# Moving the gate's work within the instruction order of ScalarE and VectorE in an attention, mixture-of-experts and dense kernel

## The reference

```
scores = x @ state.T / 8 ; xread = softmax(scores) @ state      # attention, both ways
sread  = softmax(state @ x.T / 8) @ x
x = rows of concat(xread, sread)                                # 8 * (512 + 32) = 4352 rows of 512
xn = x / (norm(x) + 1e-6) ; en = emb / (norm(emb) + 1e-6)
logits = xn @ en.T / tau ; e = argmax(logits)                   # one expert for each row
gate = softmax(logits)[e]
x = gate * (relu(x @ w1[e]) @ w2[e])
h = relu(x @ w_in) ; out = (s * h * h + b) @ w_out              # dense stage
```

## Time and profile before

| | |
|---|---|
| median of three runs | 1475.15 us |
| the profiled execution's own time | 1475.15 us |
| its span, first to last instruction | 1473.5 us |
| mean granted TensorE clock | 0.966 of full speed |
| TensorE busy | 1366.4 us, 93% |
| VectorE busy | 661.5 us, 45% |
| ScalarE busy | 511.6 us, 35% |
| GpSimd busy | 157.4 us, 11% |

### The profile page before, as it was taken

One profiled execution on the slowest core, in us unless ns is written; L12 is line 12 of the kernel. 1 busy time (PEld: TensorE's weight loads), 2 busy tenths in 40 slices (PEclk: granted clock), 3 DMA queues, 4 the chain that ended last, 5 costly groups with the idle time before them and its releaser, 6 DMA issues.

```text
span 1473.5 us, 22797 instructions
## 1 busy us (share of the span) xinstructions
PE 1366.4 (93%) x6879; PEld 1124.7 (76%) x6880; DVE 661.5 (45%) x1680; ACT 511.6 (35%) x977; POOL 157.4 (11%) x200
## 2 busy tenths in 40 slices
PE   3788668999999999998999999999999999999995
PEld 2555556888888887886888888888888888888884
DVE  2777653466765477466532322323233232422422
ACT  2555322455554355353422222222222222222221
POOL 1122220011110011015000100101001010100101
PEclk8888798999999999998999999999999999999998
DMA  8354325144423144123110000101001010010000
GB/s 218 90 123 94 73 47 187 47 172 172 172 101 115 44 171 156 61 69 125 37 43 1 29 29 0 57 0 57 0 0 57 0 57 0 23 34 0 29 0 29
DMA packets 75490, 100.21 MB, mean 68 GB/s; under 512 B 44312, under 2 KB 44856, under 8 KB 74432
## 3 DMA queue, kind: packets, MB, share of 16 engines
q1 hardware_dynamic: 62784, 69.72, 15.7%
q0 software_dynamic: 7200, 20.08, 4.1%
q10 hardware_dynamic: 5472, 9.96, 1.8%
HBM read 71.24 MB, written 28.66 MB: 68 GB/s over the span
## 4 chain that ended last, share of the span: by engine, by line
PE 80%; DVE 7%; DMA 3%; issue 3%; ACT 3%; SPq 2%; DVEq 1%; ACTq 0%; another core or an unknown queue 0%; POOL 0%; POOLq 0%
PE bank_a L1450 25%; PE bank_n L1469 13%; PE bank_t L1469 12%; PE bank_n L1403 11%; PE bank_a L1372 9%; DMA xg<-x_tok,g_idx 3%; PE bank_t L1383 2%; DVE w_lo L963 1%; PE bank_t L1190 1%; PE bank_n L1354 1%; PE bank_a L1261 1%; PE bank_n L1261 1%; PE bank_a L1173 1%; ACT x_rows L595 1%; PE bank_n L1231 1%
## 5 line engine op out<-in xcount | busy, mean ns | idle before, releaser
L1125 DVE TENSOR_TENSOR sq<-rel 128x512 f32<-128x512 f32 (+1 forms) x144 | 95.5, 663 | 487.1 <-ACT rel L764 487.1
L764 ACT ACTIVATE rel<-bank_a 128x512 f32<-128x512 f32 (+1 forms) x144 | 82.8, 575 | 541.6 <-PE bank_a L1450 541.6
L1450 PE MATMUL bank_a<-y_hi,w_in_hi 128*128 128x512 f32 (+1 forms) x576 | 217.7, 378 | 0.1
L1450 PE MATMUL bank_a<-y_hi,w_in_lo 128*128 128x512 f32 (+1 forms) x576 | 217.3, 377 | 0.0
L1450 PE MATMUL bank_a<-y_lo,w_in_hi 128*128 128x512 f32 (+1 forms) x576 | 217.3, 377 | 0.0
L1403 PE MATMUL bank_n<-w_hi,hid_hi 128*128 128x512 f32 x296 | 118.9, 402 | 16.0 <-DVE hid_lo L979 15.6
L1450 PEld LDWEIGHTS bank_a<-y_hi,w_in_hi 128*128 128x128 f32 x576 | 108.3, 188 | 21.4 <-issue 0.8
L1450 PEld LDWEIGHTS bank_a<-y_lo,w_in_hi 128*128 128x128 f32 x576 | 108.3, 188 | 20.7 <-issue 0.2
L1450 PEld LDWEIGHTS bank_a<-y_hi,w_in_lo 128*128 128x128 f32 x576 | 108.3, 188 | 19.9
L1403 PE MATMUL bank_n<-w_hi,hid_lo 128*128 128x512 f32 x296 | 117.7, 398 | 0.0
L1469 PE MATMUL bank_n<-wo_hi,g_hi 128*128 128x512 f32 x288 | 112.5, 391 | 0.7 <-DVE g_lo L1128 0.7
(11 more groups left out here) (231 smaller groups left out, 2121.2 us busy)
## 6 DMA issues: line engine op xcount, KB each, us to landing
w_raw<-in_moe_w SPq DMA_DIRECT2D x16, 2048.0 KB, 9.4
moe_tok<-yg ACTq DMA_DIRECT2D x38, 256.0 KB, 2.0
x_tok<-x_rows SPq DMA_DIRECT2D x8, 1088.0 KB
x_m<-in_x SPq DMA_DIRECT2D x8, 1024.0 KB
y_rows<-moe_tok SPq DMA_DIRECT2D x8, 1024.0 KB, 5.1
win_raw<-in_moe_w_in SPq DMA_DIRECT2D x8, 512.0 KB
w_raw<-in_moe_w_out SPq DMA_DIRECT2D x1, 4096.0 KB
slot_tab<-ids,pos POOLq DMA_INDIRECT x40
```

Source lines behind the costliest of these rows:

```text
L764: nc.scalar.activation(rel[:, k, 0:cols], ps_g[k][:, 0:cols], ACT.Relu).then_inc(rel_ready, 1)
L1125: nc.vector.tensor_tensor(sq[:, 0:cols], rel[:, k, 0:cols], rel[:, k, 0:cols], ALU.mult).then_inc(sq_ready, 1)
L1450: last = nc.tensor.matmul(ps_g[n % 2][:, 0:cols], w[:, wc], a[:, c, 0:cols], start=(c == 0 and w is w_in_hi and a is y_hi), stop=(c == DC ...
```

## The change

Only the order of calls changes. On ScalarE `gate_square(1)` is called before `hidden(0)`, `gate_soft(0)` after `next_w1(1)`, `gate_square(3)` before `hidden(2)`, `gate_square(4)` before `win_hi(0)`; in the loop `next_w1` comes before `gate_square`. On VectorE the gate of tiles 0 and 1 comes after `hidden_lo(1)`; in the loop `gate_scale` comes before `next_w1`, and `gate_logits` moves from before `next_w1` to behind `hidden_lo`.

```diff
 (scalar)
             x_hi(0)
             gate_square(0)
+            gate_square(1)
             hidden(0)
             x_hi(1)
             hidden_hi(0)
-            gate_square(1)
             hidden(1)
-            gate_soft(0)
             hidden_hi(1)
+            act.wait_ge(st_stored, 16 * B)
             act.wait_ge(tab_ready, 1)
             next_w1(1)
-            act.wait_ge(st_stored, 16 * B)
+            gate_soft(0)
             result(0)
...
             gate_soft(2)
+            gate_square(3)
             hidden(2)
             x_hi(3)
-            gate_square(3)
             next_w1(2)
             hidden_hi(2)
+            gate_square(4)
             win_hi(0)
             next_w2(1)
-            gate_square(4)
             gate_soft(3)
...
                 x_hi(g + 2)
+                next_w1(g + 1)
                 gate_square(g + 3)
-                next_w1(g + 1)
                 result(g)
 (vector)
-            gate_scale(0)
             dve.wait_ge(slot_tr, 1)
             nc.vector.tensor_copy(idx_all[:], bank_r[:, E:E + 3 * TQ]).then_inc(idx_ready, 1)
-            gate_final(0)
-            gate_scale(1)
             hidden_lo(1)
             dve.wait_ge(tab_ready, 1)
             next_w1(1)
+            gate_scale(0)
+            gate_final(0)
             x_lo(2)
             gate_logits(2)
+            gate_scale(1)
             gate_final(1)
             gate_scale(2)
+            gate_logits(3)
             gate_final(2)
             x_lo(3)
-            gate_logits(3)
+            gate_scale(3)
             next_w1(2)
             hidden_lo(2)
+            gate_logits(4)
             win_lo(0)
             next_w2(1)
-            gate_logits(4)
-            gate_scale(3)
             gate_final(3)
...
                 x_lo(g + 2)
+                gate_scale(g + 2)
+                next_w1(g + 1)
+                hidden_lo(g + 1)
                 gate_logits(g + 3)
-                next_w1(g + 1)
-                gate_scale(g + 2)
-                hidden_lo(g + 1)
                 next_w2(g)
                 gate_final(g + 2)
```

## The result

The changed kernel takes 1490.75 us (median of 4 runs, 1487.78 to 1493.85), the kernel before 1474.63 on the same chip: a ratio of 1.0108, with a 95% interval of 1.0084 to 1.0132. It is slower by 16.1 us. The forecast was 1494.

A forecast was written before the change was run, and what follows sets the result against it. TensorE, busy 93% of the span, bounds the kernel. The loop loses 17.1 us (24.3 after, 7.2 before), the start 1.0 and the last gathers 0.4: +18.5 on 1475.15, called 1494, range 1477 to 1508.

The forecast's parts named there:

- likeliest case: Whole kernel: TensorE stalls 2.0 us on the gather at six changes of expert, 1.0 more follows each; 1494 us, chance 0.50.
- VectorE's sum at a change: Loop, change of expert: gate_scale ahead of w1_lo, which ends at T + 11.9; TensorE loses about 0.9 us instead of 0.44.
- T: The end of up(g + 1) on TensorE, from which the forecast counts times in the loop.
- signs of being wrong: Profile after: no gather wait at L1354 in the loop, a w1_lo wait at L1372, or plain tiles longer than 12.25 us.
- The gather's lateness: Loop, change of expert: the gather waits for logits behind hidden_lo and is issued at T + 14.4.
- The load in its way: Loop, six changes: the gather, 2.4 us behind the w1 load, takes 7.0 us; TensorE stalls 2.0 us.
- the cover: Loop: the gather's margin before TensorE needs it, 0.45 us at worst in a plain tile, gone at a change.
- What is late next: After each of six stalls: x_lo about 0.6 us late, hidden_lo some 0.5; 1.0 us taken, bounds 0 and 1.7.
- The other bound, the clock: Behind each stall: TensorE's granted clock falls, worth 1.7 us each; as a rival 1502 us in all, chance 0.15.
- The gather under `w_out`: Last gathers, under the 4 MB load of w_out: 0.4 us lost, bounds 0 and 1.
- The start: Ahead of the loop: ScalarE waits for gather 1, up(1) comes about 2.4 us later; +1.0 us, bounds -1 and +2.
- The end of the loop: Loop's end: the gate's chain and hidden_lo keep their sum, so it costs nothing.

The follow-up runs named there:

- Experiment 6: Kernel before with only VectorE's gate_scale moved ahead of next_w1 in the loop: 1476.31 us against 1475.72, ratio 1.0016.
- experiment 4: Changed kernel with the loop's w1 loads fetching only half the rows, output wrong: 1466.78 us against 1466.59 for the kernel before, ratio 1.0001.
- experiment 1: Changed kernel with gate_logits moved back right behind x_lo in VectorE's loop: 1468.64 us against 1466.59 for the kernel before, ratio 1.0002.
- experiment 2: Kernel before with only gate_logits moved behind hidden_lo in VectorE's loop: 1482.60 us against 1466.59, ratio 1.0110.
- experiment 3: Kernel before with only the changed order of calls ahead of the loops, on both engines: 1465.76 us against 1466.59, ratio 0.9991.
- experiment 7: Kernel before with ScalarE's next_w1 ahead of gate_square and GpSimd's bias sum moved behind the last gate: 1471.98 us against 1475.72, ratio 0.9979.

## Why the prediction was right

The prediction's likeliest case came true, in its direction, its place and nearly its size.

- *VectorE's sum at a change.* Forecast: `w1_lo` ends and the w1 load goes at T + 11.95. It goes at T + 11.96. The loss of 0.9 us for it shows by itself at the seventh change: 0.96. Experiment 6 shows it is real and small. One of the signs of being wrong did come: seven waits at `up` for the last quarter of `w1_lo`, which I had ready just in time. They are 0.2 us each and lie inside the 0.96.
- *The gather's lateness.* Forecast: issue at T + 14.4 at a change. It is T + 14.16, and GpSimd's wait is put down to the logits 36 times.
- *The load in its way.* Shown: the gather takes 6.28 us, with half the load it takes no longer than with none, and the loss is gone (experiment 4); issued well ahead of the load it does no harm (experiment 1). I took 7.0 us; the six measured 6.13 to 6.30. The gather lands with the end of the load; in my sum both stood at T + 21.4, though I had the 7.0 from other rows. The 9.4 us that I took for the load is the median of a group that has the w2 loads in it as well; the w1 loads behind which the six gathers come take 8.3 to 8.7. The gather's time was 0.7 us too large and its issue 0.2 too late, so TensorE's idle time is 0.76 to 0.98 us and not 2.0.
- *What I read wrongly in the trace before.* I had today's gather out of the load's way because it is issued ahead of it. At 296.79 it is only 0.6 us ahead (the load goes at 297.40), and it is held up already. GpSimd's timeline in the trace before:

```profile
305.33 0.18 POOL L512 COPY g_idx<-idx_all 128x1 int32 x1 [7.11 <-DMA xg<-x_tok,g_idx]
```

  Its landing is seen 7.11 us after the issuing instruction's end, instead of some 3.2. It costs nothing there, since TensorE wants it only near 308 us. So the change did not bring the gather and the load together at this change of expert; it moved both later, and that used up the cover.
- *A cost that I left out.* Behind that idle time, the transposes and the start of `up` are some 0.6 to 0.8 us slower than in a row: `up` starts 0.99 us behind `turn_x` (306.53 to 307.52), 0.36 in other tiles, a third of a microsecond of it as "issue". TensorE's own register loads for the expert's number stand there, and with a full queue they would be covered; that reading of it was only argued. Idle time and this together give 1.7 us (2.67, the mean cost in the spacing over a change, less 0.96), where the forecast had 2.0. That the two come near each other is luck: the wait was taken twice too long, and the slow restart was left out.
- *What is late next.* Forecast 1.0 us a change, by `x_lo` 0.6 and `hidden_lo` 0.5. Measured 0.6 to 0.7: the next `turn_x` waits for `x_lo`, `hidden_lo` is in time. The other bound, the clock, was not reached: from 262 to 670 us, behind all six stalls, the granted clock is 1.00. That it can fall is shown in experiment 2, behind 2.9 us of waiting.
- *The gather under `w_out`.* Forecast 0.4, measured 1.4. The cover of 0.45 us is that of a plain tile, where the gather goes at T + 10.6 (284.34 with T = 273.77). This tile stands behind the w2 split of the last expert, and VectorE is late for it:

```profile
660.51 4.65 DVE L971 TENSOR_TENSOR w_lo<-w_raw,w_hi 128x1024 fp32r<-128x1024 f32 x4 [0.92 <-ACT w_hi L664]
...
672.77 1.29 DVE L979 TENSOR_TENSOR hid_lo<-bank_t,hid_hi 128x512 fp32r<-128x512 f32 x2 [1.64 <-issue]
...
675.09 0.98 POOL L519 DMA_INDIRECT xg<-x_tok,g_idx  x1 [9.89 <-DVE lgs L983]
```

  With `up` ending at 662.18 that is T + 12.9. It lands 6.33 us later, and TensorE has waited 0.64 us. The tiles behind the other w2 splits have their gathers as late (326.78 is T + 13.5), but no load in full flow beside them.
- *The start.* Forecast +1.0. In this trace it is +0.8; the four traces with the changed start have 68.4 to 71.3 us, the five with the one before 65.4 to 67.6, which would be some 3 us. The timed runs of experiment 3 show no loss. What the start costs, between nothing and 3 us, stays open. Of its parts, `up(1)` comes 2.4 us later, as forecast, and `up(2)` 1.5 later, a little outside my 1.3.
- *The end of the loop.* Forecast nothing: 803.0 and 802.5.

The sum for the loop: 6 x (0.96 + 1.7 + 0.65) + 1.0 + 1.4 = 22.3, against 24.7 in the forecast; less 7.2 that was there before. In part this too is luck, since the errors of the terms have different signs.
## What to carry to other kernels

A read that frees a single buffer belongs as early as its data allow, even when the reader's result is not needed for a long time: what hangs on it is the next transfer, not the result. When an order is changed, follow each moved read to the DMA that it frees and ask what else is in the queues at the new time; 6.7 us of lateness cost nothing in experiment 4; with the full 2 MB load in flow in front of it, or with the square ahead of the weights (experiment 2), the kernel lost 1.1%. And undo the edits one at a time: of this change one call lost 1.1%, one pair won 0.2%, and nothing else could be told from no change.

## What the runs showed of the hardware

- A gather of 128 rows of 2,176 bytes lands some 3.4 us after its issue in free queues (the median of 30 in experiment 2's trace, 3.3 to 3.9), and 6.1 to 6.3 when it is issued 2.2 us behind a 2 MB load of 8.3 to 8.7 us: it moves nothing for 4.1 us and ends with the load. Behind a load of 1 MB, issued the same 2.2 us ahead, it is not slowed at all (experiment 4). Issued 0.6 us ahead of a 2 MB load it is held up too (7.11 us behind its issuing instruction, in the trace before).
- While GpSimd adds 128 x 512 floats from SBUF, VectorE's operations L801 and L803, which write one column and read two or more from SBUF, take 1.12 to 1.30 us instead of 0.16 to 0.22; L802, which reads one column and two constants, keeps its 0.15. The held ones end where an addition ends: GpSimd's timeline has one from 684.12 for 1.26 us, to 685.38, and the L801 operation from 684.09 ends at 685.39. An operation that falls between two additions is not held (L1000 at 689.45, 0.16 us). The Trainium skill (SBUF — State Buffer, "SBUF: two separate sides") says that the two engines share a port pair which one of them holds for a whole instruction; these rows agree. Moving the sum elsewhere only moved the waits (experiment 7).
- Behind an idle time of TensorE of 0.76 to 0.98 us the granted clock stayed at 1.00, that is 2.4 GHz (changed kernel, 262 to 670 us). Behind one of 2.94 us it is 0.80 over 8.4 us, so that part of them ran at 1.2 GHz (experiment 2).
